# Single-bank transposed tiles, shared query tails and softmax inverses through DRAM in a fused attention and two-layer MoE kernel

## What is computed

```
q_rot, k_rot = rotate(q), rotate(k)                 # rotary embedding by cos, sin
scores = (q_rot @ k_rot.T) / sqrt(64)
attn = exp(scores - rowmax) ; attn = attn / (rowsum(attn) + 1e-9)
x = (attn @ v) -> rows of 2304 tokens x 512
h = x @ w1_in ;  g = s * relu(h)**2 + b      ;  x = g @ w1_out
h = x @ w2_in ;  g = h * sigmoid(1.702 * h)  ;  out = g @ w2_out
```

## Time and profile before

| what | us |
|---|---|
| median of 3 runs (lowest, highest) | 1166.18 (1165.2, 1167.83) |
| the profiled execution | 1168.41 |
| its span in the trace | 1166.6 |
| PE busy in the span | 1112.1 (95%) |
| attention, to the first feed-forward matmul | 355.5 |
| one pair of heads, PV to PV of the next | 20.3 |

### The profile page before, as it was taken

One profiled execution on the slowest core, in us unless ns is written; L12 is line 12 of the kernel. 1 busy time (PEld: TensorE's weight loads), 2 busy tenths in 40 slices (PEclk: granted clock), 3 DMA queues, 4 the chain that ended last, 5 costly groups with the idle time before them and its releaser, 6 DMA issues.

```text
span 1166.6 us, 17049 instructions
## 1 busy us (share of the span) xinstructions
PE 1112.1 (95%) x6608; PEld 1049.9 (90%) x6608; DVE 547.9 (47%) x889; ACT 512.6 (44%) x1013; POOL 238.1 (20%) x254
## 2 busy tenths in 40 slices
PE   3899999999988999999999999999999999999998
PEld 3788888888888999999999999999999999999997
DVE  3777778777765643333333335643233333323222
ACT  2777777787763542233232325542222222222222
POOL 6776867778331000000000000000000000000000
PEclk9999999999998999999999999999999999999999
DMA  6555655545313320000000003400000000000000
GB/s 137 126 122 111 142 131 122 119 111 124 72 26 103 126 71 1 1 1 1 1 1 1 1 1 98 128 29 1 28 1 15 14 1 28 1 28 1 28 1 28
DMA packets 95985, 60.60 MB, mean 52 GB/s; under 512 B 62624, under 2 KB 83232, under 8 KB 95904
## 3 DMA queue, kind: packets, MB, share of 16 engines
q1 hardware_dynamic: 95008, 59.01, 20.3%
q10 hardware_dynamic: 896, 0.49, 0.1%
HBM read 31.16 MB, written 4.72 MB: 31 GB/s over the span
## 4 chain that ended last, share of the span: by engine, by line
PE 91%; ACT 3%; issue 2%; DVE 2%; DMA 1%; POOL 1%; SPq 1%; ACTq 0%; POOLq 0%
PE psum L756 34%; PE psum L728 34%; PE psum L514 8%; PE psum L449 4%; PE psum L480 4%; PE psum L477 2%; PE psum L464 1%; PE psum L536 1%; ACT ET L560 1%; ACT QK L583 1%; DVE QK L656 1%; PE psum L526 1%; PE psum L496 1%; PE psum L534 0%; DMA wraw<-in_moe_w_out_dram 0%
## 5 line engine op out<-in xcount | busy, mean ns | idle before, releaser
L728 PE MATMUL psum<-xhi,Whi 128*128 128x384 f32 x768 | 258.5, 337 | 4.7 <-DVE Wlo L221 4.7
L728 PE MATMUL psum<-xhi,Wlo 128*128 128x384 f32 x768 | 258.4, 336 | 0.0
L728 PE MATMUL psum<-xlo,Whi 128*128 128x384 f32 x768 | 257.8, 336 | 0.0
L728 PEld LDWEIGHTS psum<-xhi,Whi 128*128 128x128 f32 x768 | 144.7, 188 | 9.2 <-DVE Wlo L221 5.0
L728 PEld LDWEIGHTS psum<-xlo,Whi 128*128 128x128 f32 x768 | 144.7, 188 | 4.1
L728 PEld LDWEIGHTS psum<-xhi,Wlo 128*128 128x128 f32 x768 | 144.6, 188 | 0.0
L885 DVE SCALAR_TENSOR_TENSOR glo<-act,sb_sb,ghi 128x384 fp32r<-128x384 f32 x96 | 59.7, 622 | 147.3 <-ACT ghi L862 147.3
L862 ACT ACTIVATE ghi<-act,sb_sb 128x384 fp32r<-128x384 f32 x96 | 59.2, 617 | 157.5 <-PE psum L756 153.6
L756 PE MATMUL psum<-ghi,Whi 128*128 128x384 f32 x384 | 128.3, 334 | 0.0
L756 PE MATMUL psum<-glo,Whi 128*128 128x384 f32 x384 | 128.3, 334 | 0.0
L756 PE MATMUL psum<-ghi,Wlo 128*128 128x384 f32 x384 | 128.3, 334 | 0.0
(11 more groups left out here) (92 smaller groups left out, 1855.9 us busy)
## 6 DMA issues: line engine op xcount, KB each, us to landing
Q<-QK SPq DMA_DIRECT2D x64, 144.0 KB, 2.5
QK<-QK SPq DMA_DIRECT2D x32, 288.0 KB, 3.3
wraw<-in_moe_w_in_dram SPq DMA_DIRECT2D x32, 256.0 KB, 2.8
wraw<-in_moe_w_out_dram SPq DMA_DIRECT2D x32, 256.0 KB, 3.1
rest<-O SPq DMA_DIRECT2D x32, 144.0 KB, 2.3
raw<-in_q_dram SPq DMA_DIRECT2D x32, 128.0 KB, 3.0
raw<-in_k_dram SPq DMA_DIRECT2D x32, 128.0 KB, 2.5
vraw<-in_v_dram SPq DMA_DIRECT2D x32, 128.0 KB, 2.4
```

The lines of the kernel that those rows point to most:

```text
L728: mm = pe.matmul(hps(n), w[i][:, kt * P:(kt + 1) * P], x[C % 2][:, kt, :], start=kt == 0 and j == 0, stop=kt == KT - 1 and j == 2)
```

## The change

- X tiles hold the 512 main queries only, four transposes in one bank of PSUM. The tail queries of both heads get a tile of their own, **XQ**: four transposes a pair, one bank, split by **hiQ** (ACT) and **loQ** (DVE) with a permuted access pattern. `Xhi` and `Xlo` become one tensor each with a head dimension.
- PSUM is tracked by bank: X and XQ take one of eight banks, all other jobs two.
- The last tile of PV of head 1 is in three pieces (22 matmuls instead of 20).
- evac copies only the 64 rows that are wanted; the add is on DVE (**sum**, function `total`), reads the other 64 rows straight from PSUM, and writes `osum`, now double. The rest copies on SP and add on POOL are gone. PV's space comes free at the sum, not at the evac.
- widen and B are gone. The 128 x 9 inverses are written to DRAM in transposed order (**put**), and read back as a row repeated over 64 partitions for each head, in three transfers (**get**). finish is one instruction on POOL, 128 x 576.
- The first two weight tiles are split on POOL, one after step 14 and one after step 15, each once `rotated`, `prep_t` (and for the second `v_lo`) allow it.
- All five orders and the placement in PSUM are new.

```
-    PE_ORDER = order("S12@0 prep0@2 S13@0 X00@0 X01@0 S00@1 S01@1 ST@1 prep1@2 S02@1 S03@1 X02@0 X03@0 S10@1 PV1@-1 "
-                     "X10@0 X11@0 XT@0 X12@0 X13@0 B@-1 S11@1 PV0@0")
...
-    DVE_ORDER = order("max01@0 lo01@-1 maxT@0 max02@0 klo1@1 max03@0 max10@0 lo02@-1 lo03@-1 lo10@-1 lo11@-1 loT@-1 "
-                      "lo12@-1 inv@-1 max11@0 lo13@-1 finish@-2 max12@0 klo0@2 max13@0 lo00@0 max00@1")
-    POOL_ORDER = order("V0@0 add0@-1 vlo0@0 rot0@3 rot1@3 V1@0 add1@-1 vlo1@0")
-    SP_ORDER = order("loadv1@-3 loadv0@-2 load1@0 qcopy1@-1 kcopy0@-1 rest1@-4 kcopy1@-1 load0@1 rest0@-3 qcopy0@0")
+    PE_ORDER = order("S01@1 X00@0 S02@1 X01@0 S03@1 prep1@2 S10@1 S11@1 S12@1 X02@0 X03@0 S13@1 ST@1 PV1@-1 XQ@0 XT@0 "
+                     "X10@0 prep0@3 X11@0 X12@0 X13@0 S00@2 PV0@0")
+    ACT_ORDER = order("hi03@-1 evac1@-2 hiQ@-1 hiT@-1 qk0@2 hi10@-1 hi11@-1 hi12@-1 hi13@-1 exp00@1 evac0@-1 hi00@0 "
+                      "exp01@1 hi01@0 exp02@1 qk1@2 exp03@1 exp10@1 exp11@1 exp12@1 hi02@0 exp13@1 expT@1")
+    DVE_ORDER = order("lo00@0 max03@1 lo01@0 klo1@2 max10@1 max11@1 max12@1 inv@0 max13@1 maxT@1 lo02@0 lo03@0 sum1@-1 "
+                      "loQ@0 loT@0 klo0@3 lo10@0 lo11@0 max00@2 lo12@0 lo13@0 max01@2 sum0@0 max02@2")
+    POOL_ORDER = order("vlo0@0 finish@-2 V1@0 rot1@3 vlo1@0 rot0@4 V0@1")
+    SP_ORDER = order("qcopy0@0 load1@1 kcopy0@0 loadv0@-2 qcopy1@0 loadv1@-2 put@-2 kcopy1@0 get@-3 load0@2")
+    SLOTS = [3, 3, 0, 2, 2, 3, 0, 1, 2, 7, 6, 0, 1, 2, 1, 1, 0, 2, 6, 7, 1, 1, 2]
+    BANK_ORDER = (2, 3, 0, 6, 7, 1, 4, 5)
...
+    def banks_of(kind, h, j):
+        slot = SLOT[(kind, h, j)]
+        return (slot,) if kind in ("X", "XQ") else (2 * slot, 2 * slot + 1)
...
             elif kind == "PV":
-                need(eng, evac_done, 2 * p + h + 1)
+                need(eng, sum_done, 2 * p + h + 1)
...
+        def first_w(pool, s, zero):
+            i = s - (NPAIR - 2)
+            if 0 <= i < AHEAD:
+                pool.wait_ge(wraw_in[i], 32)
+                pool.wait_ge(rotated, 2 * NPAIR - 1)
+                pool.wait_ge(prep_t, 2 * NPAIR)
+                if i == 1:
+                    pool.wait_ge(v_lo, 2 * NPAIR)
+                pool.tensor_tensor(Whi[i][:], wraw[:, i, :], zero[:, :].broadcast_to([P, 2 * DM]), ALU.add).then_inc(w_hi_done, 1)
+                split_w(pool, i, False)
...
+                def put_inv(p, _, __):
+                    sp.wait_ge(inv_done, p + 1)
+                    need(sp, inv_in[p % 2], 48 * (p // 2))
+                    sp.dma_start(inv_dram[p % 2].rearrange("t p -> p t"), inv[p % 2][:], allow_slow_non_contiguous=True).then_inc(inv_out[p % 2], 16)
+
+                def get_inv(p, _, __):
+                    sp.wait_ge(inv_out[p % 2], 16 * (p // 2 + 1))
+                    need(sp, x_done, p)
+                    flat = inv_dram[p % 2].rearrange("t p -> (t p)")
+                    for h, at, a, n in ((0, 0, 0, S), (1, 0, S + TAIL, MAIN), (1, MAIN, S, TAIL)):
+                        sp.dma_start(inv_row[rows_of(h), at:at + n],
+                                     flat[a:a + n].rearrange("(o q) -> o q", o=1).to_broadcast([D, n])).then_inc(inv_in[p % 2], 16)
...
+                def finish(p, _, __):
+                    b, t = p // KT * S, p % KT
+                    pool.wait_ge(sum_done, 2 * p + 2)
+                    pool.wait_ge(inv_in[p % 2], 48 * (p // 2 + 1))
+                    pool.tensor_tensor(xT[:, t, b:b + S], osum[p % 2][:], inv_row[:], ALU.mult).then_inc(x_done, 1)
...
-                    pe.transpose(ps[:, at:at + P], ET[p % 2][:, j * P:(j + 1) * P], id_sb[:])
-                    c = h * TAIL + j * P
+                    ps, c = banks("X", h, j), h * TAIL + j * P
                     for t in range(NM):
-                        mm = pe.transpose(ps[:, r + t * P:r + (t + 1) * P], E[p % 2][:, t, h, c:c + P], id_sb[:])
+                        mm = pe.transpose(ps[:, t * P:(t + 1) * P], E[p % 2][:, t, h, c:c + P], id_sb[:])
                     mm.then_inc(x_t, 1)
+
+                def XQ_job(p, _, __):
...
+                    for j in range(NM):
+                        mm = pe.transpose(ps[:, j * P:(j + 1) * P], ET[p % 2][:, j * P:(j + 1) * P], id_sb[:])
+                    mm.then_inc(xQ_t, 1)
...
+                        pieces = PIECES[0] if j < NM or h == 0 else (PIECES[0][0], (BANK, r + MAIN, BANK - r), (r + MAIN, r + S, -TAIL))
...
-                def B_job(p, _, __):
...
-                    need(act, added, 2 * (p - 1) + h + 1)
-                    act.copy(O[h][:], row(banks("PV", h), h)).then_inc(evac_done, 1)
+                    need(act, sum_done, 2 * (p - 1) + h + 1)
+                    r = rows_of(h)
+                    act.copy(O[r, :], row(banks("PV", h), 0)[r, :]).then_inc(evac_done, 1)
...
+                def total(p, h, _):
+
+                    dve.wait_ge(evac_done, 2 * p + h + 1)
+                    if h == 0:
+                        need(dve, x_done, p - 1)
+                    r = rows_of(h)
+                    dve.tensor_tensor(osum[p % 2][r, :], row(banks("PV", h), 0)[rows_of(1 - h), :], O[r, :], ALU.add).then_inc(sum_done, 1)
```

More of the change, by code:

```diff
@@ L280, in fused_kernel @@
             sums_eps = sb("sums_eps", [P, 2 * NM + 1])
[L282 to L286, removed]
+            O = sb("O", [P, S])
+            osum = [sb(f"osum{i}", [P, S]) for i in range(2)]
+            inv = [sb(f"inv{i}", [P, 2 * NM + 1]) for i in range(2)]
+            inv_row = sb("inv_row", [P, S])
+            inv_dram = [nc.dram_tensor(f"inv_dram{i}", [2 * NM + 1, P], F32, kind="Internal").ap() for i in range(2)]
             q_h = q.rearrange("b h s d -> (b h) s d")
@@ L377, in attention_sync @@
                 sp.dma_start(sb_sb[:, 1:2], w_b.rearrange("(a b) -> a b", a=1).to_broadcast([P, 1])).then_inc(sb_in, 16)
-                program(SP_ORDER, {"load": load, "loadv": load_next_v, "qcopy": q_copies, "kcopy": k_copy, "rest": load_rest}, after)
+                program(SP_ORDER, {"load": load, "loadv": load_next_v, "qcopy": q_copies, "kcopy": k_copy, "put": put_inv, "get": get_inv}, after)
             def attention_gpsimd(pool):
@@ L409, in lo_V @@
                     pool.tensor_tensor(V[h][:, :, 1 - h, :], vraw[:, h, :, :], V[h][:, :, h, :].bitcast(F32), ALU.subtract).then_inc(v_lo, 1)
[L410 to L423, removed]
[L424 to L427 removed]
+                def finish(p, _, __):
[3 more added lines that the diff above has]
+                    pool.tensor_tensor(xT[:, t, b:b + S], osum[p % 2][:], inv_row[:], ALU.mult).then_inc(x_done, 1)
                 pool.wait_ge(tabs_in, 96)
                 def after(s):
[L432 to L436 removed]
+                    first_x(pool, s - 1, False)
+                    first_w(pool, s, zero)
+                program(POOL_ORDER, {"rot": rotate_one, "V": hi_V, "vlo": lo_V, "finish": finish}, after)
             def attention_tensor(pe):
@@ L566, in hi, with hiQ @@
                         need(act, pv_done, 2 * (p - 1) + h + 1)
-                    act.copy(Xhi[h][:, j, :], row(banks("X", h, j), h)).then_inc(et_hi, 1)
+                    act.copy(Xhi[:, h, j, 0:MAIN], banks("X", h, j)).then_inc(et_hi, 1)
+                def hiQ(p, _, __):
+                    act.wait_ge(xQ_t, p + 1)
+                    need(act, pv_done, 2 * p)
+                    act.copy(Xhi[:, :, :, MAIN:S], by_heads(banks("XQ"))).then_inc(etQ_hi, 1)
                 def hiT(p, _, __):
@@ L601, in after @@
                     first_x(act, s, True)
-                    first_w(act, s, True)
-                program(ACT_ORDER, {"exp": exp, "expT": expT, "hi": hi, "hiT": hiT, "evac": evac, "qk": qk, "widen": widen},
+                program(ACT_ORDER, {"exp": exp, "expT": expT, "hi": hi, "hiQ": hiQ, "hiT": hiT, "evac": evac, "qk": qk},
                         after)
@@ L668, in attention_vector @@
                 dve.wait_ge(scale_set, 1)
-                program(DVE_ORDER, {"max": rowmax, "maxT": rowmaxT, "lo": lo, "loT": loT, "inv": invert, "finish": finish,
-                                    "klo": qk_low}, lambda s: first_w(dve, s - 1, False))
-                return finish_pair
+                program(DVE_ORDER, {"max": rowmax, "maxT": rowmaxT, "lo": lo, "loQ": loQ, "loT": loT, "inv": invert, "sum": total,
+                                    "klo": qk_low})
         with ExitStack() as ctx:
```

151 lines of the change are left out of this document (54 added, 97 removed).

## The result

The changed kernel takes 1188.1 us (median of 4 runs, 1184.45 to 1189.17), the kernel before 1165.69 in the same series (4 runs, 1164.54 to 1167.83): a ratio of 1.0185, with 1.0158 to 1.0211 as its 95% interval. It is 22 us slower, where I had forecast 30 faster. The profiled execution took 1184.45 us, its span is 1182.6.

What follows compares the result with a forecast made beforehand. PE was taken to bound the attention stage, loosely. Savings of 22.8 (periods), 1 (start), 5 (turn) and 1.3 (weight tile 2) make 30 us: 1168.4 to 1138.4 profiled, 1136 for the median; range 1124 to 1158.

Steps and rivals of the forecast that it cites:

- the price of put: Put's write to DRAM, per pair: 1152 elements at 40 ns each, 2.9 us of every DMA engine.
- The estimate of 1.8 us: Alternative price of put from the skill's factor of 19: 1.5 ns an element, 1.8 us instead of 2.9.
- the room behind it: SP's queue behind put: kcopy1 and load0 have over 10 us until S10 and rot0 need them.
- The slower rival: Put's packets bind DMA: from 131 ns an element they set the period; at 150 ns 1179 us. Chance 0.10.
- My sign for it: Sign of being wrong: DMA share of 0.8 or more, with S10 or rot waiting on DMA.
- Period: Attention, PV0 to PV0 per pair: 18.6 us instead of 20.23, bounds 18.1 and 19.1; 22.8 us saved over 14.
- the walk: One step of the new orders: PE waits 1.6 us on 16.5, giving a period of 18.1.
- Start: Start of attention: PV0 of pair 0 ends about 1 us earlier; bounds 3 later and 3 earlier.
- Turn: From PV0 of pair 14 to the first feed-forward product: 16.3 us instead of 21.3, saving 5; bounds 2 and 7.
- Weight tile 2: Feed-forward start: PE's wait for a low weight part falls from 4.7 to about 3.4 us, saving 1.3; bounds 0 and 3.
- Sum: Whole kernel: savings 22.8 + 1 + 5 + 1.3 = 30 us, from 1168.4 to 1138.4 for the profiled execution.
- DVE: DVE per pair: net +0.3, about 15.8 us; two sums at 0.67 each; lost overlap about 0.3 us.

Runs made afterwards that it cites:

- the spread put: The changed kernel with put writing its 1152 4-byte elements each 512 bytes apart and the gets reading the identity table: 1145.07 us.
- the run with the blocks: The changed kernel with inverses transposed in 32x32 blocks on DVE and put as four DMAs of nine 128-byte runs: 1144.75 us, ratio 0.981 to the kernel before.

## Why the prediction was wrong

**The step that failed is the price of put**: "1152 x 40 / 16 = 2.9 us of every DMA engine", with "Bounds: zero, and nothing in the trace above 40". The runs show 9.0 to 12.3 us for one put where SP waits for it, 10.6 in the mean, with next to nothing else moving, and a median of 11.7 in the kernel before; shared over 16 engines the 10.6 are 10.6 x 16 / 1152 = 147 ns an element. I had taken the mean packet of a queue of loads and copies for a kind of write that no row showed, and set it as the upper bound. "Nothing above 40" said only that the trace had no such write, and 40 is a mean, which some packets of the trace must be above. The gap was wider than the prediction had it, too: the mean packet has 621 bytes (59.01 MB / 95008), some 155 times the 4 bytes of an element and not sixty. The estimate of 1.8 us, from the factor of 19 in the Trainium skill's VectorE: DVE Perf Modes, "The three transpose paths", is low by about six times here; that section ties the loss to a large destination stride, and the runs go the other way: elements 512 bytes apart and more land in 2.9 us, neighbours in one row in 9.0 to 12.3. The descriptor for each element (the Trainium skill, DMA: Bandwidth & Descriptors, "Rules for kernel authors") is there in the packets, 114976 for the 96288 of the run without a put, and is free by the spread put.

**The second failure is the room behind it**: kcopy1 and load0 "have over 10 us until S10 and rot0 need them". For kcopy1 it was close (PE stood 3.4 us). For load0 it was wrong in kind. I walked PE, DVE and ACT through a step of the new orders, but not SP and POOL, and so missed the loop finish, get, load0, rot0, V, finish. With landings of 3 us it takes about 16 us (my estimate from the lengths of its rows), under PE's 19, and is silent: in the run with the blocks rot0 waits for a load for 1.9 us at most from 60 to 300 us, where the changed kernel has 8.9. With a held stretch inside it takes 22.7. Without get's issues it takes about 20 and the put costs 9 us; with them, 42.

**The slower rival was the right one**, at 0.10: "at 150 ns ... 1179", where some 147 ns and 1188 were measured. Its price was right and its mechanism holds in part, so that the nearness of 1179 is in part luck. I had it as bandwidth, a DMA share of 0.8 or more with the copies setting the period; in truth the share falls to 0.00, and the latency in the loop sets the period. My sign for it would have been looked for in the wrong direction. That put's landing "within 6 us" would show me right did serve: it is 9.0 to 12.3.

**What held**, by the run with the blocks, whose profiled execution stands 24.5 us under that of before (1168.4 less 1143.87) where the sum said 30. By medians it is 21.4 (1166.13 less 1144.75): 3 of the 24.5 are the place of the two profiled executions among their runs.
- Period: 19.0 us for most pairs (the chain's starts of PV0 from 49.62 to 182.71, seven periods), 18.9 over all 14 (313.82 less 49.62, over 14). Forecast 18.6, bounds 18.1 and 19.1. 14 x (20.23 - 18.88) = 18.9 saved for 22.8. The first waits are those of the walk: 0.24 us for sum0 at S03 (forecast 0.2), 0.40 for exp02 at S10 (0.5). The steady period is 0.4 above the forecast, by terms that no run takes apart.
- Start: PV0 of pair 0 ends at 52.42, 1.8 later than the 50.66 of before (1.6 by the ends of PV0 in both), where I had it 1 earlier; inside the bounds, 2.8 off.
- Turn: from the end of PV0 of pair 14 (316.74) to the first product (331.63) 14.9 us; forecast 16.3, before 21.3. 6.4 saved for 5. The product itself comes 1.6 us behind the 322 to 330 that I gave as a sign, by the later start and the longer periods.
- Weight tile 2: PE waits 4.0 us for 4.7; forecast 3.4. The last gets wait for finish behind the second split on POOL, as forecast, and the third weight load is issued only at 334.36.
- Sum: 18.9 - 1.8 + 6.4 + 0.7 = 24.2, the 24.5 of the profile. The range of 1124 to 1158 would have held it.
- DVE: sum has 0.755 us, as a lo of 576 columns had (0.75), so its length is as forecast. The overlap is lost around it, as the Trainium skill's VectorE: DVE Perf Modes, "Two Vector instructions with no wait between them", had led me to expect, and the trace agrees: behind each of the 25 sums from 60 to 300 us the next instruction starts 0.03 to 0.04 us after sum's end, where two others of DVE mostly overlap by 0.07 to 0.09. That is 0.11 at each border, so up to 0.4 a pair for the 0.3 named. The permuted reads of hiQ and loQ are free (586 and 692 ns beside 593 and 680).

## What to carry to other kernels

A DMA whose kind is in no row has no upper bound from the mean packet of its queue: price it by a run of its own. Look at who writes next to whom in DRAM, and if many partitions each write 4 bytes of one row, write longer runs (36 bytes were enough here) or turn the data on an engine first (a block transpose of 0.21 us and 36 runs of 128 bytes did for 1152 scattered writes of 4 bytes). When a wait is added in front of a load on a queue, walk the loop through that queue and the engine that frees its buffers as well as the compute engines; its sum of latencies is a period like any other. A DMA share that fell to 0.00 behind an issue, with transfers outstanding, was here a held path and not an idle one.

## What the hardware did that I had not expected

- 1152 writes of 4 bytes into nine rows of 512 bytes take 9.0 to 12.3 us to land, and the 16 DMA engines move almost nothing for 8 us of it in the changed kernel, for up to 11 where nothing else is issued; with 384 into three rows it is 6 to 7, with 128 into one row about 5. The same 1152 at 512 bytes apart land in 2.9 us, runs of 36 or 128 bytes do no harm. Whether the unit that is shared is 512 bytes or a smaller one was not tried, nor whether reads of that kind do the same.
- It does not matter which queue issues them: 1188 us from SP's, 1186 from ACT's.
- Issues of other DMAs on SP can get long in the held stretch: the three gets took 5.0 and 5.75 us in two of eleven pairs, and 1.7 to 2.1 in the others.
- The profile's own books mislead here: some 35 ns an element in the changed kernel, 260 with a third of the put, and a share of 0.00 for eleven microseconds in a row.
